# A linear-attention recurrence fused with two MLPs: attention in steps of all eight heads with 64-token chunks

## The chip, the core and the metric

One core of a Trainium2 chip runs the whole program. The metric is the device time of one execution in microseconds, the median of several runs. Engines are named as in the profile: PE is TensorE, DVE is VectorE, ACT is ScalarE, POOL is GpSimd, SP is SyncE, which here only starts DMAs.

## What is computed

A recurrence over 768 tokens with a decaying 48 x 48 state for each of 4 batches and 8 heads, then two MLPs on the 3072 resulting tokens: 384 to 2048 and back, first with an ELU, then with a sigmoid-gated unit.

```python
for t in range(S):                       # B, H, S, D = 4, 8, 768, 48
    cur = np.einsum('bhd,bhe->bhde', u[None] * kt, vt)
    y[:, :, t] = np.einsum('bhd,bhde->bhe', rt, state + cur)
    state = wt[:, :, :, None] * state + np.einsum('bhd,bhe->bhde', kt, vt)
x = y.transpose(0, 2, 1, 3).reshape(B * S, H * D)
h = x @ w_in;  x = where(h > 0, h, exp(min(h, 0)) - 1) @ w_out
h = x @ w2_in; out = (h / (1 + exp(-1.702 * h))) @ w2_out
```

## The kernel before

**The recurrence by levels.** Instead of going token by token, the kernel takes chunks of 128 tokens. Inside a chunk, the score of two tokens needs the product of all decays between them. It is built by halving: at level h (1, 2, 4 ... 64) the right half of each block of 2h tokens in r and the left half in k are multiplied by decays (`update`, lines 545 to 558, DVE), and PE multiplies k by r for the pairs whose nearest common block has that size (`products`, line 748). The decays of blocks come from a tree of products (`tree`, line 528). For small h the matmuls compute 32 x 32 blocks, more than is needed, and DVE picks the wanted entries through masks (`pick`, line 576, L596). The scores of the token with itself come from u*k (here u*r, `near`, line 734). Between chunks there is a state: k is transposed by PE (`turn_products`, L114), multiplied by v (`kv_products`, L127), and DVE carries the state (`state_update`, L154). The outputs y are scores times v (L137) plus state times r (L143), accumulated in PSUM.

**Steps.** A step treats half a sequence (384 tokens, `HALF`) of four heads (`U` = 2 pairs; the two heads of a pair lie on partitions 0 to 47 and 64 to 111). Eight heads, two halves and four batches give 16 steps, indexed (i, x). The end of a step (turning k, states, outputs) is done inside the next step. Everything is double buffered in x.

**The MLP rides.** A group is 384 tokens through one MLP; there are 8 groups for each MLP. A group has 16 hidden tiles of 128, and each tile takes nine matmuls up (`up`, L824) and nine down (`down`, L842), 128 x 128 on 384 columns, because fp32 numbers are split into a high and a low part in fp32r (x_hi, x_lo; g_hi, g_lo; the two halves of a weight tile), and three of the four products are kept. The last 13 of the 16 steps (`LAG` = 3) each carry half a group: eight up blocks, then eight down pieces. After each up block ACT computes relu and exp (L423, L425), DVE the gate (L620), ACT its high part (L429), DVE its low part (L625). The order of the work on every engine is written out by hand in a `step` function for each engine; for PE it alternates:

```python
level(i, x, half, 0, 1, first)      # attention: one level of one pair of heads
mlp(3)                              # MLP: nine matmuls
```

**Data paths.** SP loads r, k, w, u of a step (`load`, line 265), stores y to `y_scratch` in HBM (`store`, L297) and reads a full group of x back from it (`load_x`, L308), which ACT and DVE split (L436, L644). The first six results of the first MLP go to `x2_scratch` in HBM. During the first steps, the weights of MLP 1 arrive through two staging buffers, ACT copies the high part (L416) and POOL computes the low part (L351).

**The second part.** `mlps` (line 874) holds the last step's end, the rest of MLP 1 (one and a half groups) and the 8 groups of MLP 2, in which up and down alternate tile by tile (L1201, L1212). The weights of MLP 2 replace those of MLP 1 tile by tile.

## Time and profile before

| | |
|---|---|
| median of 3 runs | 1101.1 us (1100.88 to 1101.79) |
| the profiled execution | 1101.46 us |
| its span, first to last instruction | 1099.3 us |
| PE / PE weight loads / DVE / ACT / POOL busy | 94% / 87% / 59% / 44% / 7% |
| granted TensorE clock, mean | 0.975 |
| HBM read, written | 39.96 MB, 12.98 MB |

The span is shorter than the time of its execution by what lies around the first and the last instruction. A busy share is that of an engine over the whole span. In the timeline a burst of like instructions is one row with its count, its start and the time from its first start to its last end; a matmul's record lasts longer than the distance to the next one's start, since matmuls overlap. An fp32 matmul leaves two records, an fp32r matmul and a transpose one. The granted clock is a share of 2.4 GHz; 0.5 is 1.2 GHz.

### The profile page before, as it was taken

The page shows a single profiled execution, that of the slowest core. Times are in us where ns is not written, and L with a number is a line of the kernel's source. Part 1 is how long each engine was busy: PE and PEld are TensorE (multiplying, and loading weights), DVE is VectorE, ACT ScalarE, POOL GpSimd, SP SyncE. Part 2 cuts the span into 40 slices and gives each one's busy share as a digit, 9 for nine tenths or more (in the row PEclk, how much of TensorE's full clock was granted, in tenths as well). Part 3 has the DMA queues.
Part 4 walks back from the last instruction along what each step waited for, and adds up shares of the span by engine and source line. Part 5 has one row for each costly group of instructions (what it writes and reads, how often), then busy time and mean ns, then how long its engine had stood idle before and what let it go on. Part 6 is the DMA issues. An engine that isn't in the chain of part 4 may idle for free. (4 is left out here: it accounts for less than half of the span.)

```text
span 1099.3 us, 27196 instructions
## 1 busy us (share of the span) xinstructions
PE 1033.3 (94%) x10912; PEld 951.5 (87%) x10912; DVE 645.0 (59%) x1587; ACT 488.2 (44%) x987; POOL 73.3 (7%) x55
## 2 busy tenths in 40 slices
PE   2658999999899999999999999999999999999998
PEld 1547888888788888788888899999999999999998
DVE  7998677677577687477676543333443434343433
ACT  2445455446246445346444457633333333333332
POOL 5450000000000000000000006400000000000000
PEclk9758999999999999999999999999999999999999
DMA  7453212212212212212210413200000000000000
GB/s 167 106 142 78 49 43 65 56 45 55 58 45 56 56 45 66 46 45 61 51 47 33 146 60 115 73 1 22 1 21 0 21 22 0 21 0 22 1 22 22
DMA packets 24096, 54.56 MB, mean 50 GB/s; under 512 B 3248, under 2 KB 15792, under 8 KB 23984
## 3 DMA queue, kind: packets, MB, share of 16 engines
q1 hardware_dynamic: 22704, 46.66, 16.4%
q0 software_dynamic: 1280, 6.29, 2.0%
q8 instruction: 84, 1.38, 0.6%
q14 instruction: 28, 0.23, 0.1%
HBM read 39.96 MB, written 12.98 MB: 48 GB/s over the span
## 5 line engine op out<-in xcount | busy, mean ns | idle before, releaser
L1201 PE MATMUL psum<-x_hi,w_split 128*128 128x384 f32 x912 | 232.6, 336 | 0.0
L1212 PE MATMUL psum<-g_hi,w_split 128*128 128x384 f32 x912 | 232.6, 336 | 0.0
L842 PE MATMUL psum<-g_hi,w_split 128*128 128x384 f32 x624 | 172.5, 348 | 0.0
L1119 DVE TENSOR_TENSOR gate<-expo,psum 128x384 f32<-128x384 f32 x128 | 70.9, 554 | 160.6 <-ACT expo L1038 160.6
L1201 PEld LDWEIGHTS psum<-x_hi,w_split 128*128 128x128 f32 x912 | 164.9, 188 | 0.0
L1212 PEld LDWEIGHTS psum<-g_hi,w_split 128*128 128x128 f32 x912 | 164.8, 188 | 0.0
L824 PE MATMUL psum<-x_hi,w_split 128*128 128x384 f32 x624 | 161.3, 340 | 0.0
L1201 PE MATMUL psum<-x_lo,w_split 128*128 128x384 f32 x456 | 153.5, 337 | 0.1
L1212 PE MATMUL psum<-g_lo,w_split 128*128 128x384 f32 x456 | 153.3, 336 | 0.0
L1038 ACT ACTIVATE expo<-psum 128x384 f32<-128x384 f32 x128 | 63.0, 492 | 170.4 <-PE psum L1201 170.4
L1125 DVE TENSOR_TENSOR g_lo<-gate,g_hi 128x384 fp32r<-128x384 f32 x152 | 84.9, 559 | 90.2 <-ACT g_hi L1045 90.2
L824 PE MATMUL psum<-x_lo,w_split 128*128 128x384 f32 x312 | 116.7, 374 | 8.2 <-DVE gate L620 6.2
L1045 ACT ACTIVATE g_hi<-gate 128x384 fp32r<-128x384 f32 x152 | 80.1, 527 | 97.9 <-DVE gate L1119 82.4
L556 DVE TENSOR_TENSOR raw<-raw,wtree 128x384 f32<-128x384 f32 x160 | 96.6, 604 | 40.5 <-PE psum L765 32.4
L842 PEld LDWEIGHTS psum<-g_hi,w_split 128*128 128x128 f32 x624 | 111.8, 188 | 5.9 <-issue 2.2
L824 PEld LDWEIGHTS psum<-x_hi,w_split 128*128 128x128 f32 x624 | 115.0, 191 | 0.0
L620 DVE SCALAR_TENSOR_TENSOR gate<-expo,psum 128x384 f32<-128x384 f32 x104 | 57.7, 554 | 86.9 <-ACT expo L425 85.5
L842 PE MATMUL psum<-g_lo,w_split 128*128 128x384 f32 x312 | 107.8, 346 | 0.0
L429 ACT ACTIVATE g_hi<-gate 128x384 fp32r<-128x384 f32 x104 | 54.8, 527 | 84.7 <-DVE gate L620 84.7
L759 PEld LDWEIGHTS psum<-raw 128*32 128x32 f32 (+1 forms) x3840 | 50.1, 115 | 43.6 <-issue 43.6
L1201 PEld LDWEIGHTS psum<-x_lo,w_split 128*128 128x128 f32 x456 | 85.6, 188 | 0.6 <-DVE x_lo L1113 0.4
L1212 PEld LDWEIGHTS psum<-g_lo,w_split 128*128 128x128 f32 x456 | 85.6, 188 | 0.0
(85 smaller groups left out, 1222.5 us busy)
## 6 DMA issues: line engine op xcount, KB each, us to landing
raw<-rkwu_dram SPq DMA_DIRECT2D x32, 288.4 KB, 5.7
staging<-weights_dram POOLq DMA_DIRECT2D x16, 384.0 KB, 3.9
raw<-rkwu_dram SPq DMA_DIRECT2D x32, 144.0 KB, 4.5
v_sb<-v_tokens_dram SPq DMA_DIRECT2D x16, 288.0 KB, 2.8
y_scratch<-y_sb SPq DMA_DIRECT2D x64, 72.0 KB, 1.8
staging<-y_scratch SPq DMA_DIRECT2D x7, 576.0 KB, 4.5
out_dram<-o_sb SPq DMA_DIRECT2D x7, 576.0 KB, 3.0
x_scratch<-x_sb SPq DMA_DIRECT2D x6, 576.0 KB, 3.3
```

The lines of the kernel that those rows point to most:

```text
L429: act.activation(g_hi[:, f, :], gate[:, :], ACT.Copy).then_inc(hi_done, 1)
L556: dve.tensor_tensor(r, r, wr, ALU.mult).then_inc(upd_done, 1)
L620: dve.scalar_tensor_tensor(out=gate[:, :], in0=expo[:, :], scalar=-1.0, in1=mlp_bank(f, x), op0=ALU.add, op1=ALU.max).then_inc(gate_done, 1)
L759: mm = pe.matmul(dst.rearrange("p (a b h) -> p a b h", a=2, h=h), kk[:, o:o + m], right_half(r[:, :, o:o + 32], h), start=True, stop=True)
L824: mm = pe.matmul(mlp_bank(f, x), w_tile((1 - x) * FT + f, lo, kt * P), xx, start=n == 0, stop=n == 3 * KT - 1)
L842: mm = pe.matmul(mlp_bank(FT + m, x), w_tile((1 - x) * FT + f, lo, (KT + m) * P), gg[:, f, :], start=at == 0, stop=at == 3 * FT - 1)
L1038: act.activation(expo[:, f % 2, :], hidden(f), ACT.Sigmoid, scale=1.702).then_inc(exp_done, 1)
L1045: act.activation(g_hi[:, f % 4, :], gate[:, f % 2, :], ACT.Copy).then_inc(hi_done, 1)
L1119: dve.tensor_tensor(gate[:, f % 2, :], expo[:, f % 2, :], hidden(f), ALU.mult).then_inc(gate_done, 1)
L1125: dve.tensor_tensor(g_lo[:, f % 4, :], gate[:, f % 2, :], g_hi[:, f % 4, :].bitcast(F32), ALU.subtract).then_inc(lo_done, 1)
L1201: mm = pe.matmul(hidden(f), w_tile(f, lo, kt * P), xx, start=n == 0, stop=n == 3 * KT - 1)
L1212: mm = pe.matmul(acc(q, m), w_tile(f, lo, (KT + m) * P), gg, start=f == first_tile(g) and n == 0, stop=f == NF - 1 and n == 2)
```

## The change

The attention is written anew, and both parts become one program.

- A step holds all eight heads (`U` = 4 pairs) of half a sequence; there are 8 steps instead of 16. A step's own end (turning, states, outputs) lies in the step itself.
- Chunks have 64 tokens (`CH`), so level 64 goes away and there are 6 chunks in a half instead of 3.
- Each level is one burst on PE for all heads and one pair of updates on DVE (1536 and 768 elements a partition). Only step 0 works in two halves (`grow_pair`).
- The bonus u multiplies k (`bonus`, ACT).
- Keys-values and outputs use 64 rows of the array (a chunk's tokens) or 48, and turn from matmul to matmul through both halves of the rows and of the columns.
- Steps 1 to 7 each carry a full group of MLP 1 (16 tiles), up and down alternating as in the second part. Step 0 carries none. Group 7 of MLP 1 and MLP 2 follow as before.
- x of a group is put together in SBUF (`x_raw`): PSUM goes to it and to `y3` by copies, and six small DMAs from SBUF to SBUF (`fill_gaps`, three on SP, three on POOL) move rows of heads 6 and 7 into the partitions 48 to 63 and 112 to 127. The rows of w_in are reordered on the host to match. `y_scratch` is gone.
- r, k, w and v have one buffer each, the next step's being loaded as soon as this step is through with each. MLP 1's weights use three staging buffers, and DVE computes their low parts in step 0 (`w1_low`); POOL does so only for MLP 2.

```diff
-CH = 128
-U = 2
-LAG = 3
+U = H // 2
+CH = 64
+NC = T // CH
+NB = T // P
...
+                def load_rv(i):
+                    sp.wait_ge(y_done, (i - 1) * N_Y + N_Y)
+                    for a, src in enumerate(of_step(r_dram, i)):
+                        sp.dma_start(arena[64 * a:64 * a + D, a * UT:(a + 1) * UT], src).then_inc(r_in, 16)
+                    sp.dma_start(v_sb[:].rearrange("p c u a e -> p (c u a e)"),
+                                 v_dram[bass.ds(i, 1)].rearrange("o s n -> (o s) n")).then_inc(v_in, 16)
+                def fill_gaps(i):
+                    sp.wait_ge(xc_done, i * N_XC + N_XC)
+                    sp.wait_ge(yc_done, i * N_YC + N_YC)
+                    for m in range(KT):
+                        sp.dma_start(x_raw[48:64, m, :], y3[16 * m:16 * m + 16, 0, :]).then_inc(gap_sp, 16)
...
+                def step(i, stored=None, more=True):
+                    if stored is not None:
+                        store_x2(stored)
+                    if more:
+                        load_w(i + 1)
+                        load_k(i + 1)
+                    fill_gaps(i)
+                    if more:
+                        load_rv(i + 1)
...
+                def load(f):
+                    pool.dma_start(w1_raw[f % NW1], weights1[f]).then_inc(w1_in[f % NW1], 16)
...
+                for f in range(NW1, 11):
+                    pool.wait_ge(wlo_done, f - NW1 + 1)
+                    load(f)
+                fill_gaps(0)
+                for f in range(11, NF):
+                    pool.wait_ge(wlo_done, f - NW1 + 1)
+                    load(f)
+                with pool.Fori(1, STEPS) as i:
+                    fill_gaps(i)
...
+                def update_r(i, k, us):
+                    h = 1 << (k - 1)
+                    d = decay(k, us)
+                    n = d.shape[1]
+                    z = r[:, :, us, :].rearrange("p a u (b two h) -> p a (u b) two h", two=2, h=h)[:, :, :, 1, :]
+                    by = d[:, :, 0:1].rearrange("p (o b) one -> p o b one", o=1).to_broadcast([P, 2, n, h])
+                    return dve.tensor_tensor(z, z, by, ALU.mult)
...
+                def grow_r(i, k):
+                    open_update(i, k, 1)
+                    if k > 1:
+                        dve.wait_ge(upd_done, upd(i, k - 1, 1))
+                    update_r(i, k, ALL).then_inc(upd_done, 1)
+                def grow_k(i, k):
+                    update_k(i, k, ALL).then_inc(upd_done, 1)
+                def grow_pair(k, pair):
+                    open_update(0, k, pair)
+                    if k > 1:
+                        dve.wait_ge(upd_done, upd(0, k - 1, pair))
+                    us = slice(2 * pair, 2 * pair + 2)
+                    update_r(0, k, us)
+                    update_k(0, k, us).then_inc(upd_done, 1)
...
+                def pick(i, h):
+                    k = NEAR.index(h)
+                    dve.wait_ge(lev_done, lev(i, k, 1))
+                    if h == 1:
+                        dve.wait_ge(pick_done, i * N_PICK + 2)
+                    else:
+                        dve.wait_ge(pick_done, i * N_PICK + PICKS[h] - 1)
+                    dve.sem_inc(pick_open, 1)
+                    src = BANKS[(k + 2) % 3][:, 0:384]
+                    m = masks[:, M_OFF[h]:M_OFF[h] + 16].rearrange("p (o b h) -> p o b h", o=1, h=h).to_broadcast(
+                        [P, 24, 16 // h, h])
...
+                def w1_low(f):
+                    dve.wait_ge(whi_done, f + 1)
+                    at = 2 * f * WF
+                    dve.tensor_tensor(w_split[:, at + WF:at + 2 * WF], w1_raw[f % NW1],
+                                      w_split[:, at:at + WF].bitcast(F32), ALU.subtract).then_inc(wlo_done, 1)
...
+                def near(i):
...
+                        if first:
+                            pe.wait_ge(uk_done, 2 * pair + 2)
+                        for u in (2 * pair, 2 * pair + 1):
+                            for c in range(NB):
+                                for j in range(4):
+                                    o = c * P + 32 * j
+                                    at = (u % 2) * 192 + c * 64
+                                    pe.matmul(BANKS[pair][32 * j:32 * j + 32, at:at + 64].rearrange("p (a t) -> p a t", a=2),
+                                              uk[:, u, o:o + 32], r[:, :, u, o:o + 32], start=True, stop=True)
+                        products(1, Z, pair).then_inc(lev_done, 1)
...
+                def products(h, bank, pair):
...
+                                for par in range(2):
+                                    o = c * P + 64 * par
+                                    to = 64 * par + 32 * pair
+                                    mm = pe.matmul(bank[to:to + 32, at:at + 64].rearrange("p (a t) -> p a t", a=2),
+                                                   kk[:, u, o:o + 32], r[:, :, u, o + 32:o + 64], start=True, stop=True)
+                    return mm
+                def level(i, k):
+                    if k < 5:
+                        pe.wait_ge(pick_done, i * N_PICK + k)
+                    else:
+                        pe.wait_ge(pick_done, i * N_PICK + PICKS[4])
+                    split = type(i) is int and i == 0
+                    for pair in range(2):
+                        if split:
+                            pe.wait_ge(upd_done, upd(i, k, pair))
+                        elif pair == 0:
+                            pe.wait_ge(upd_done, upd(i, k, 1))
+                        if split or pair == 0:
+                            pe.sem_inc(level_open, 1)
+                        products(1 << k, BANKS[(k + 2) % 3] if k < 5 else Y, pair).then_inc(lev_done, 1)
...
+                def keys_values(i, half):
+                    def product(c, u, a):
+                        z, slot = PLACE[c]
+                        rows = slice(64 * (c % 2), 64 * (c % 2) + 64)
+                        at = (slot + u) * D
+                        n = (u * NB + c // 2) * P + 64 * a
+                        return pe.matmul(BANKS[z][64 * a:64 * a + 64, at:at + D], kt[rows, n:n + 64],
+                                         v_sb[rows, c // 2, u, a, :], start=True, stop=True)
...
+                    pe.sem_inc(level_open, 1)
+                    for even in (0, 2):
+                        for u in range(U):
+                            for a in range(2):
+                                product(even, u, a)
+                                mm = product(even + 1, u, a)
+                    mm.then_inc(kv_done, 1)
+                    for u in range(U):
+                        for a in range(2):
+                            mm = product(4, u, a)
+                    mm.then_inc(kv_done, 1 + half)
+                    if half == 0:
+                        pe.wait_ge(kv_done, i * N_KV + 2)
+                        pe.sem_inc(level_open, 1)
+                        for u in range(U):
+                            for a in range(2):
+                                mm = product(5, u, a)
+                        mm.then_inc(kv_done, 1)
...
+                def outputs(b, i, half):
+                    def place(c, u, a):
+                        z, slot = PLACE[c]
+                        to = 64 * (a ^ (u % 2))
+                        at = (slot + u) * CH
+                        return BANKS[z][to:to + D, at:at + CH]
+                    def from_scores(c, u, a):
+                        rows = slice(64 * (c % 2), 64 * (c % 2) + 64)
+                        return pe.matmul(place(c, u, a), v_sb[rows, c // 2, u, a, :], scores[rows, u, c // 2, a, :],
+                                         start=c in (0, 1, 4) and u == 0, stop=False, skip_group_check=True)
+                    def from_state(c, u, a):
+                        rows = slice(64 * a, 64 * a + D)
+                        return pe.matmul(place(c, u, a), state[rows, (c - 1) % NC, u, :],
+                                         r[rows, a, u, c * CH:(c + 1) * CH], start=False, stop=True, skip_group_check=True)
+                    pe.wait_ge(asm_done, i * N_ASM + N_ASM)
+                    pe.wait_ge(state_done, states_before(b, half) + N_STATE[half])
+                    pe.sem_inc(level_open, 1)
+                    for n, pair in enumerate(((4, 1), (0, 3), (2, 5))):
+                        if n == 2:
+                            pe.wait_ge(y_done, i * N_Y + 1)
+                            pe.sem_inc(level_open, 1)
+                        for u in range(U):
+                            for a in range(2):
+                                for c in pair:
+                                    mm = from_scores(c, u, a)
+                        if n != 1:
+                            mm.then_inc(y_done, 1)
+                    for n, (even, odd) in enumerate((((0, 2), (1, 3)), ((4, 5), (0, 2)), ((1, 3), (4, 5)))):
+                        pe.wait_ge(y_done, i * N_Y + 2 + n)
+                        pe.sem_inc(level_open, 1)
+                        for u in range(0, U, 2):
+                            for z in range(2):
+                                for c, uu in ((even[z], u), (odd[z], u + 1)):
+                                    if half == 1 or c > 0:
+                                        for a in range(2):
+                                            mm = from_state(c, uu, a)
+                        mm.then_inc(y_done, 1)
...
+                def step(b, i, half, g, q, more=True):
+                    def unit_up(f):
+                        if f + 2 < NF:
+                            up(g, q, f + 2)
+                        else:
+                            up(g + 1, 1 - q, f + 2 - NF)
+                    def unit_down(f):
+                        down(g, f, 0, freed=f == 0 and (type(g) is not int or g > 0))
+                    def unit(f):
+                        unit_up(f)
+                        unit_down(f)
+                    unit_up(0)
+                    level(i, 1)
+                    unit_down(0)
+                    unit(1)
+                    level(i, 2)
+                    unit(2)
+                    unit_up(3)
+                    level(i, 3)
+                    unit_down(3)
+                    unit(4)
+                    level(i, 4)
+                    unit(5)
+                    unit_up(6)
+                    level(i, 5)
+                    unit_down(6)
+                    unit(7)
+                    turn(i)
+                    unit(8)
+                    unit_up(9)
+                    keys_values(i, half)
+                    unit_down(9)
+                    unit(10)
+                    unit_up(11)
+                    outputs(b, i, half)
+                    unit_down(11)
+                    unit(12)
+                    unit(13)
+                    unit(14)
+                    if more:
+                        near(i + 1)
+                    unit(15)
```

On PE, around a level of a riding step before (`raw` holds r and k):

```order
L824 MATMUL psum<-x_hi,w_split 128x384 x2
L759 MATMUL psum<-raw 32x32 x12
L824 MATMUL psum<-x_lo,w_split 128x384
L824 MATMUL psum<-x_hi,w_split 128x384 x2
L824 MATMUL psum<-x_lo,w_split 128x384
L824 MATMUL psum<-x_hi,w_split 128x384 x2
L824 MATMUL psum<-x_lo,w_split 128x384
L824 MATMUL psum<-x_hi,w_split 128x384 x2
L114 MATMUL psum<-ident,k_fin 128x128 x3
L759 MATMUL psum<-raw 32x32 x12
```

and now (`arena` holds r and k, and more):

```order
L964 MATMUL psum<-x_lo,w_split 128x384
L964 MATMUL psum<-x_hi,w_split 128x384 x2
L832 MATMUL psum<-arena 32x32 x48
L977 MATMUL psum<-g_lo,w_split 128x384
L977 MATMUL psum<-g_hi,w_split 128x384 x2
L977 MATMUL psum<-g_lo,w_split 128x384
L977 MATMUL psum<-g_hi,w_split 128x384 x2
L977 MATMUL psum<-g_lo,w_split 128x384
```

Before, 12 matmuls of one pair of heads stand behind a block of nine MLP matmuls; now 48 of all heads stand in one piece, with 18 to 27 MLP matmuls to the next level.

On DVE, in a riding step, before (`raw<-raw,wtree` are updates, `gate` and `g_lo` the MLP's, `scores<-diag` the end of the step before):

```order
L620 SCALAR_TENSOR_TENSOR gate<-expo,psum 128x384
L556 TENSOR_TENSOR raw<-raw,wtree_2 128x192x2
L558 TENSOR_TENSOR raw<-raw,wtree_2 128x96x2
L625 TENSOR_TENSOR g_lo<-gate,g_hi 128x384
L603 COPY scores<-diag 32x6x32 x4
L620 SCALAR_TENSOR_TENSOR gate<-expo,psum 128x384
L154 SCALAR_TENSOR_TENSOR state<-state,wchunk,psum 128x48 x4
L556 TENSOR_TENSOR raw<-raw,wtree_4 128x96x4
```

and now, from the update of level 3 to the update of level 4 (shapes are strided, 384x4 and 192x8 both make 1536 elements with the two heads):

```order
L533 TENSOR_TENSOR arena<-arena 128x384x4
L627 SCALAR_TENSOR_TENSOR gate<-expo,psum 128x384
L539 TENSOR_TENSOR arena<-arena 128x192x4
L632 TENSOR_TENSOR g_lo<-gate,g_hi 128x384
L584 COPY_PREDICATED blocks<-masks,psum 128x384
L627 SCALAR_TENSOR_TENSOR gate<-expo,psum 128x384
L533 TENSOR_TENSOR arena<-arena 128x192x8
L632 TENSOR_TENSOR g_lo<-gate,g_hi 128x384
```

The picks, which stood together at the end of a step, now stand between the levels, one behind each update of k, and the levels after them wait for them.

On SP, in a step of before with its x:

```order
L279 DMA raw<-rkwu_dram 48x2x384
L281 DMA raw<-rkwu_dram 48x1538
L279 DMA raw<-rkwu_dram 48x2x384
L281 DMA raw<-rkwu_dram 48x1538
L297 DMA y_scratch<-y_sb 48x384 x4
L285 DMA v_sb<-v_tokens_dram 128x576
L308 DMA staging<-y_scratch 128x3x384
```

and now:

```order
L171 DMA arena<-w_channels_dram 48x1536 x2
L171 DMA arena<-k_channels_dram 48x1536 x2
L198 DMA x_raw<-y 16x384 x3
L189 DMA arena<-r_channels_dram 48x1536 x2
L190 DMA v_sb<-v_tokens_dram 128x1152
```

The loads of r and v stand behind the three DMAs that fill x_raw, and those behind the loads of w and k.

## Rows read from the trace of the kernel before

**Rows 1.** The page: parts 1 and 2, busy time and the 40 slices.
```profile
PE 1033.3 (94%) x10912; PEld 951.5 (87%) x10912; DVE 645.0 (59%) x1587; ACT 488.2 (44%) x987; POOL 73.3 (7%) x55
...
PE   2658999999899999999999999999999999999998
```

**Rows 2.** The windows: busy us (instructions) of each engine, granted clock, DMA share, GB/s.
```profile
0.00:95.00 95.00, 47.03 (x1116) 37.27 (x1117) 83.10 (x183) 35.31 (x64) 43.13 (x39) 0.75 0.54 133
95.00:615.30 520.30, 505.38 (x6994) 435.28 (x6994) 368.63 (x1059) 257.47 (x557) 0.00 (x0) 0.99 0.22 51
3.00:13.00 10.00, 0.00 (x0) 0.00 (x0) 4.35 (x7) 0.95 (x2) 1.97 (x3) 1.00 0.93 217
298.00:299.00 1.00, 1.00 (x8) 1.00 (x5) 0.54 (x2) 0.00 (x0) 0.00 (x0) 0.73 0.07 16
```

**Rows 3.** The chain of waits, last stage: start us, length us, what.
```profile
893.26 1.57 PE psum L1201 x9
```

**Rows 4.** The timeline of PE, riding steps: start us, length us, engine, line, what, count.
```profile
134.33 0.54 PE L744 MATMUL psum<-ur,raw 128*32 128x64 f32 x24
134.69 0.37 PE L759 MATMUL psum<-raw 128*32 128x32 f32 x24
134.99 0.45 PE L824 MATMUL psum<-x_lo,w_split 128*128 128x384 f32 x1
...
303.55 0.45 PE L824 MATMUL psum<-x_lo,w_split 128*128 128x384 f32 x1
...
305.26 0.49 PE L114 MATMUL psum<-ident,k_fin 128*128 128x128 f32 x3
...
312.57 0.86 PE L137 MATMUL psum<-scores,v_sb 128*48 128x128 f32 x12
313.37 0.86 PE L143 MATMUL psum<-r_fin,state 48*48 48x128 f32 x12
...
324.92 0.53 PE L765 MATMUL psum<-raw 128*32 128x64 f32 x12
325.38 0.44 PE L842 MATMUL psum<-g_hi,w_split 128*128 128x384 f32 x1
```

**Rows 5.** The timeline of PE before the riding steps, at half clock.
```profile
86.23 0.81 PE L759 MATMUL psum<-raw 128*32 128x32 f32 x48
```

**Rows 6.** The timeline of PE: a step's first row, and the loop's edge.
```profile
251.67 0.54 PE L744 MATMUL psum<-ur,raw 128*32 128x64 f32 x24
...
292.56 0.54 PE L744 MATMUL psum<-ur,raw 128*32 128x64 f32 x24 [1.09 <-issue]
...
297.45 0.36 PE L744 MATMUL psum<-ur,raw 128*32 128x64 f32 x10 [2.03 <-issue]
```

**Rows 7.** The timeline of DVE in a riding step.
```profile
107.00 0.55 DVE L556 TENSOR_TENSOR raw<-raw,wtree 128x384 f32<-128x384 f32 x1
107.47 0.35 DVE L558 TENSOR_TENSOR raw<-raw,wtree 128x192 f32<-128x192 f32 x1
107.74 0.55 DVE L625 TENSOR_TENSOR g_lo<-gate,g_hi 128x384 fp32r<-128x384 f32 x1
```

**Rows 8.** The DMA issues: KB each, median us from issue to landing.
```profile
raw<-rkwu_dram SPq DMA_DIRECT2D x32, 288.4 KB, 5.7
staging<-weights_dram POOLq DMA_DIRECT2D x16, 384.0 KB, 3.9
...
y_scratch<-y_sb SPq DMA_DIRECT2D x64, 72.0 KB, 1.8
```

**Rows 9.** The waits of PE: us in total, times, longest us.
```profile
PE psum L824 <- DVE gate L620: 6.2, 12, 0.6
...
PE psum L824 <- DVE x_lo L644: 2.0, 6, 0.4
```

**Rows 10.** The timeline of DVE and POOL in the start.
```profile
22.10 2.03 POOL L351 TENSOR_TENSOR w_split<-staging,w_split 128x768 fp32r<-128x768 f32 x1 [2.72 <-ACT w_split L416]
...
22.37 2.17 DVE L556 TENSOR_TENSOR raw<-raw,wtree 128x384 f32<-128x384 f32 x1
```

1700 lines of the change are left out of this document (707 added, 993 removed).

## Prediction

> **What bounds the kernel now.** I read the page first [rows 1]: PE is busy for 94% of the span, its loads for 87%, DVE for 59%. Only the first four of the 40 slices fall short on PE; from the fifth on every digit but the last is 9. So the time is what PE has to do, plus the start. The windows divide it [rows 2]: 95.0 us before the first MLP matmul (PE busy 47.0 of them, granted clock 0.75), 520.3 us in which MLP and attention share PE, and the last 484.0 us of MLP. In the last stage the chain of waits consists of PE pieces, nine matmuls in 1.56 to 1.57 us [rows 3]: 0.1737 us for one, and no engine is waited for. All 4608 MLP matmuls (16 groups, 16 tiles, 18 each) come to 4608 x 0.1737 = 800.4 us. They are the same in both kernels, so only 1099.3 - 800.4 = 298.9 us can be argued about: the start, the attention's own matmuls, waits and the two ends.
>
> The timeline of a riding step gives the rates [rows 4]. Every fp32 matmul leaves two records, so L744's 12 matmuls stand as x24. From the start of a burst to the next: L744 0.36 us; L759 0.30; L137 0.80; L765 0.46. The MLP block behind a burst runs from 303.55 to 305.26, 1.71 us where 1.56 would do: re-entry costs 0.15. The L759 burst of 134.69 ends at 135.06 and one record lasts 0.205 (mean), so its last start is 134.86: 24 starts in 0.17 us, 7 ns each, and the other 0.14 of its 0.30 is draining. A burst is thus about 0.15 fixed, plus columns: L744 (64 columns, four column groups at once) 13 to 15 ns a record; L765 (64 columns, two groups) (0.46 - 0.15)/12 = 26; L137 (128 columns, two groups) (0.80 - 0.15)/12 = 54. All fit one rule: time goes with columns and falls with the number of groups at work. At half clock, 48 records of L759 take 0.81 [rows 5], (0.81 - 0.205)/47 = 13 ns, twice as much.
>
> **The riding steps.** Three steps of before lie between the L744 bursts at 134.33 and 251.67 [rows 4, 6]: 39.1 us each, 25.0 of it MLP; two of them, 78.2 us, do what one new step does. The new step has 288 MLP matmuls, 50.0 us, and these bursts:
> near, 48 matmuls of L744's kind and 48 of L759's: 96 x 14 + 96 x 8 ns + 0.15 = 2.3 us. Levels 1 to 4, 96 records at 8 ns + 0.15 = 0.92 each, 3.7. Level 5 (32 x 64, two groups): 48 x 26 ns + 0.15 = 1.4. Level 6 of before (L769) is gone, since chunks are 64 tokens. Twelve transposes of 128 columns, one record each, 54 ns: 0.8. Keys and values, 40 or 48 matmuls of 48 columns: 20 ns a record with two groups, by L765's rate; here both halves of the rows and of the columns are used in turn, 10 ns if four quadrants work at once: 1.3 with the second wait. Outputs, 88 to 96 matmuls of 64 columns: 184 x 13 ns + five waits for its own last result at 0.25 = 3.7. Re-entry nine times, where before has some 34 in two steps: 1.35. Sum 14.6.
> Four quadrants at once is a choice: no row of before shows it (L143 uses two, on the diagonal, at L137's pace). I take it since the rate went down with each further part of the array in use. The other bound is two, 20 and 27 ns: 3.4 us more a step. The Trainium skill, TensorEngine Tiling (Array Packing), Available Configurations, lists 64x64 as four independent tiles; that would be my value, and no run here shows it yet.
>
> Waits. DVE costs come from start to start [rows 7]: 128x384 0.47, 128x192 0.27, so about 0.06 + 1.07 ns an element; the 1536-element update 1.7, its k part 0.88, together 2.6 a level for all heads. A pick of 384 I put at the same 0.5. A step holds 16 x 0.95 for the gates, 15.5 for updates, 3.5 for picks, 4.4 for states, 1.3 for the split and 4 of the rest: 44 of 67 us. It fits, but each level has its own deadline. Laying both orders against each other, with elu 1.1 us after `up` and a level 0.92: level 3 waits for pick(1) (DVE through at 16.6 us, PE there at 16.2) 0.4; level 5 for pick(4) 0.4; transposes for pick(16) 0.35; outputs for the last states 0.5. The rest of the MLP hides the remainder, 1.5 to 2 units of 3.13 us between levels. `up` of the next group waits for x_lo: after the outputs come the copies 0.9, DMAs from SBUF to SBUF (y_scratch's 72 KB landed in 1.8 [rows 8]; POOL takes 0.56 to issue one), ACT's split 1.15, DVE's tree and split 3.3: 8.8 us, against five MLP blocks, 7.8: 1.0. r of the next step, queued on SP behind the gap DMAs, lands some 8 us after the outputs (5.7 [rows 8]), and `near` comes after 11: hidden, by 3 us. Together 2.75, all after waits that before had too (gate 6.2 us in 12, x_lo 2.0 in 6 [rows 9]). Between nothing and 6 us a step is possible.
> A step: 50.0 + 14.6 + 2.75 = 67.4, against 78.2.
>
> **The start.** Before's is bound by DVE, and by POOL beside it: when POOL splits a weight tile (2.03 us), one DVE operation of 0.55 lasts 2.17 [rows 10]; 16 such tiles cost DVE some 26 us. Now DVE does that work itself, 16 x 0.86 = 13.8, and POOL computes nothing. But only one step runs ahead of the MLP, not three. By the clock: 217 GB/s flowed from 3 to 13 us [rows 2], so 1.8 MB of k, r, w is there at 13; tree 2.5; six levels of two pairs 24 with picks, three weight tiles and waits, 39.7. Then the weights bind: three buffers, a reload 0.56 + 3.9 [rows 8] + 0.84 on ACT: w1_low(7) ends at 50.6; states 55.2; outputs at half clock 61.7; copies, gaps, and r with v behind them 69.7; near 3.8 at half clock, updates and split 77.4; the last eight weight tiles through three buffers, two reload rounds deep, 91.5. `up(0, 2)` starts at about 92. The y_scratch round trips go; they were hidden, and I cost them at nothing.
>
> **The sum.** 92 + 4590 x 0.1737 (797.3; 18 matmuls are done before) + 7 x 14.6 less one near (99.8) + 7 x 2.75 (19.3) + one loop edge + 2 for the clock after PE's idle time + 3.5 at the end. The edge: at before's, PE idles 1.09 and again 2.03 us in the midst of L744, with nothing to wait for, and the granted clock is 0.73 in the microsecond behind [rows 2, 6]; two steps grow by 5.4. The new loop has one such edge. 1019.3 us of span. The profiled execution took 1101.46 for a span of 1099.3, 2.2 more, and the median is 0.4 below it: 1021.
>
> **Rivals.** (A) **Two quadrants only**: 7 x 3.4 = 24 more, 1045. For it: before never has row halves at work in one column group. Chance 0.17.
> (B) **Small matmuls keep a price**: a level costs four times its old piece, 1.28, and near 2.64, since nothing longer than 48 records of this kind is in the trace; the 7 ns could be a queue filled beforehand. 4 x 0.36 + 0.5 = 1.9 a step, 13 in all; with A, 1058. Against it: the 48 records at half clock kept half the rate [rows 5]. The Trainium skill, the same page, Instruction Overhead, says a matmul has about 60 cycles of overhead, so that one of few columns lasts as long as one of 60. By that, L759 would cost what L744 does, 14 ns, and a level 1.5: 1036. The rows speak against it (7 ns against 13 to 15). Chance 0.10, A's part aside.
> (C) **DVE's deadlines**: all six levels, kv, outputs and near each 0.7 us later: 6.3 a step, 44 in all, 1065. For it: bursts cannot start before all heads' updates are through, where before's first pair hid the second's. Against: 44 of 67 us busy. Chance 0.10.
> (D) **Slower: instructions run short.** A burst of near is 384 instructions (records and their loads) in 2.2 us, outputs 370 in 3.7; before's longest is 96 at that rate. Where PE ran dry behind the loop edge it lost 2.03 us, and with the clock's drop 3.7 in that step. If that happens in bursts as such: 63 bursts; from 22 of them on (80/3.7) the kernel is slower than before; in half of them 32 x 3.7 = 118, 1139. Against it: 18 MLP matmuls, 36 instructions in 3.13 us, stand between most bursts and leave the fetch time, and PE shows no such hole away from the loop's edge [rows 1]. Chance 0.05.
> (E) **No change in what matters**: the new step has 460 attention matmuls for two times 197, so with A, B and C together PE gains nothing from bursts: 78 a step, 7 x 10.6 = 74 more, 1095. Chance 0.03; half of that within 0.2%.
>
> **The numbers.** The forecast, 1021, has 0.55. A, B, C reach to 1065. The start may be 8 us off to either side, the stalls nothing (19 less): about 1000 below. Range 1000 to 1062 leaves out D, E, and a little of C and of the lower end. A measurement here tells 0.2% from no change. Faster 0.93, within 0.2% 0.02, slower 0.05.
>
> **What would show it.** Right: near to near in a steady step 66 to 69 us; a level of 96 records in 0.8 to 1.0; outputs 3.5 to 4; `up(0, 2)` at 85 to 98; DVE operations in the start at their own length; PE idle before levels 3 and 5 under 1 us each. Wrong: level bursts of 1.3 (B), outputs above 5.5 (A), idle time of PE put down to issue inside bursts (D), or PE waiting for DVE more than 5 us a step (C).

## The result, and the profile after

The changed kernel takes 1057.6 us (median of four runs, 1055.5 to 1058.4) where the kernel before takes 1101.2: ratio 0.9601, 95% interval 0.9586 to 0.9616. It is faster, inside the range of 1000 to 1062, and 36.6 us slower than the forecast of 1021. The profiled execution took 1057.42 with a span of 1055.4, so the 2.0 us around the span are as assumed (2.2), and the miss lies in the span: 1055.4 against 1019.3. One execution of a kernel further down, that with seven staging buffers, took 1568.7 us at a granted clock of 0.56, and is left out of that kernel's ratio as slow.

The page of the changed kernel, parts 1 and 2, answers to [rows 1]:

```profile
PE 953.0 (90%) x11872; PEld 922.3 (87%) x11872; DVE 546.2 (52%) x894; ACT 456.8 (43%) x859; POOL 56.5 (5%) x65
...
PE   2434999998998988999999999999999999999998
```

PE is 80 us less busy (1033.3 before), although it executes more instructions, and its share fell from 94% to 90%. The work shrank as meant; what the forecast lacked is in idle time. Four slices of the riding steps show an 8. The windows cut the span where the terms of the sum end (columns as in rows 2: busy us and count of PE, PE's loads, DVE, ACT, POOL; clock; DMA share; GB/s):

```profile
0.00:101.48 101.48, 35.47 (x1119) 32.09 (x1119) 54.24 (x83) 29.23 (x45) 16.23 (x28) 0.97 0.45 118
101.48:530.92 429.44, 398.84 (x6966) 375.30 (x6966) 269.10 (x430) 214.27 (x413) 8.68 (x18) 0.99 0.18 43
530.92:1055.40 524.48, 518.67 (x3789) 514.94 (x3788) 222.85 (x382) 213.34 (x402) 31.62 (x19) 1.00 0.09 32
```

`up(0, 2)` starts at 101.48 and not at 92: 9.5 of the 36.1 us. Behind it come 953.9 us instead of 927.3: 26.6 more, some 23 of them before 530.92, where PE is idle for 30.6 us, and the rest in the seventh riding step behind it. The waits of PE between 102 and 560 us, and the one that is over by 101.48 (us in total, times, longest):

```profile
PE psum L964 <- DVE gate L627: 11.4, 2, 10.3
PE psum L964 <- DVE x_lo L614: 8.0, 6, 1.5
PE psum L832 <- DVE blocks L584: 6.9, 7, 1.0
PE psum L964 <- issue: 3.8, 5, 0.9
PE psum L841 <- DVE blocks L584: 3.3, 6, 0.6
PE psum L977 <- issue: 2.1, 2, 1.0
...
PE psum L832 <- issue: 1.4, 2, 0.8
PE psum L872 <- DVE blocks L584: 1.3, 6, 0.2
```

Two kinds stand there: DVE's deadlines (x_lo, and the picks of L584), some 19.5 us; and 7.3 us of "issue" in L964, L977 and L832, for which the forecast had 5.4 at one loop edge.

One straight step, the one whose `near` starts at 460.28, from PE's timeline, answers to [rows 4]:

```profile
460.28 0.88 PE L819 MATMUL psum<-arena 128*32 128x64 f32 x48
...
486.22 1.02 PE L832 MATMUL psum<-arena 128*16 128x32 f32 x96
...
492.63 0.58 PE L841 MATMUL psum<-arena 128*32 128x64 f32 x14 [0.49 <-DVE blocks L584]
...
498.72 0.60 PE L872 MATMUL psum<-ident,arena 128*128 128x128 f32 x4
499.54 0.66 PE L872 MATMUL psum<-ident,arena 128*128 128x128 f32 x4 [0.22 <-DVE blocks L584]
...
505.27 1.61 PE L884 MATMUL psum<-v_sb,arena 64*64 64x48 f32 x80
...
507.63 0.44 PE L977 MATMUL psum<-g_lo,w_split 128*128 128x384 f32 x1
...
514.26 1.56 PE L918 MATMUL psum<-blocks,v_sb 64*48 64x64 f32 x96
516.01 1.45 PE L923 MATMUL psum<-arena,state 48*48 48x64 f32 x48 [0.19 <-PE psum L918]
...
518.24 0.44 PE L977 MATMUL psum<-g_lo,w_split 128*128 128x384 f32 x1
...
527.60 0.44 PE L964 MATMUL psum<-x_lo,w_split 128*128 128x384 f32 x1 [1.25 <-DVE x_lo L614]
...
530.92 0.77 PE L819 MATMUL psum<-arena 128*32 128x64 f32 x40
```

It takes 70.64 us; 67.4 was forecast. From start to start, less the waits, beside the forecast's terms: `near` 2.31 (2.3); levels 1 to 4, of which L832 at 486.22 is one (0.95), 3.94 (3.7); level 5 1.28 (1.4); transposes 1.45 (0.8); keys and values 507.63 - 505.27 = 2.36 (1.3); outputs 3.98 (3.7); the MLP's own 50.0. The blocks of 27 MLP matmuls between the bursts last 4.8 to 4.9 us where 27 x 0.1737 is 4.69, so re-entries come to 2.4 (1.35); waits 0.93, 0.49, 0.22 and 1.25, together 2.9 (2.75, whose own five terms make 2.65). The excesses, 0.24 - 0.12 + 0.65 + 1.06 + 0.28 + 1.05 + 0.15, make 3.3, which is the miss (3.24 from start to start) but for rounding.

That step is in straight code behind PE's loop. The loop's own four start at 167.76, 238.88, 312.58 and 386.72 and took 71.12, 73.70, 74.14 and 73.56: three of the four are 3 us longer. In the first of these three PE's timeline has three holes in the midst of MLP pieces:

```profile
243.10 0.62 PE L964 MATMUL psum<-x_hi,w_split 128*128 128x384 f32 x2 [0.95 <-issue]
...
250.48 0.34 PE L977 MATMUL psum<-g_hi,w_split 128*128 128x384 f32 x1 [1.04 <-issue]
...
265.17 0.51 PE L964 MATMUL psum<-x_hi,w_split 128*128 128x384 f32 x2 [0.76 <-issue]
```

The same three matmuls of the loop's second pass, 147.7 us later, have holes of 0.77, 1.04 and 0.77.

Ratios below are to the kernel before, run on the same chip; where an experiment is compared with the changed kernel, it is by the difference of its ratio to 0.9601, times 1101.2 us. With the intervals of the ratios, such a difference is good to some 3 to 4 us either way, so the bursts and waits in the timelines are read beside it.

### The profile page after: what moved, and what is told of

The parts are those of the page before. It is cut to its first block, busy times and chain, and to the rows that moved or that the text cites. A ratio compares the mean times of both kernels' runs of the same rounds, so it can differ in the third digit from the quotient of the medians.

```text
span 1055.4 us, 27022 instructions
## 1 busy us (share of the span) xinstructions
PE 953.0 (90%) x11872; PEld 922.3 (87%) x11872; DVE 546.2 (52%) x894; ACT 456.8 (43%) x859; POOL 56.5 (5%) x65
## 3 DMA queue, kind: packets, MB, share of 16 engines
q1 hardware_dynamic: 12448, 38.74, 13.5%
q8 instruction: 87, 1.43, 0.6%
## 4 chain that ended last, share of the span: by engine, by line
PE 79%; DVE 7%; issue 3%; ACT 3%; DMA 1%; SPq 0%; DVEq 0%; POOL 0%; POOLq 0%
PE psum L964 36%; PE psum L977 33%; PE psum L832 3%; ACT expo L363 1%; PE psum L923 1%; DVE blocks L584 1%; ACT expo L361 1%; DVE arena L515 1%; PE psum L884 1%; PE psum L819 1%; PE psum L918 1%; DVE gate L627 1%; DVE arena L539 1%; PE psum L841 1%; DVE x_lo L614 1%
## 5 line engine op out<-in xcount | busy, mean ns | idle before, releaser
L964 PE MATMUL psum<-x_hi,w_split 128*128 128x384 f32 x1536 | 396.1, 339 | 3.2 <-issue 3.2
L977 PE MATMUL psum<-g_hi,w_split 128*128 128x384 f32 x1536 | 391.3, 336 | 2.1 <-issue 2.1
L964 PE MATMUL psum<-x_lo,w_split 128*128 128x384 f32 x768 | 264.8, 345 | 24.1 <-DVE x_lo L614 12.0
L964 PEld LDWEIGHTS psum<-x_hi,w_split 128*128 128x128 f32 x1536 | 281.9, 189 | 5.1 <-issue 4.9
L977 PEld LDWEIGHTS psum<-g_hi,w_split 128*128 128x128 f32 x1536 | 277.0, 188 | 0.0
L977 PE MATMUL psum<-g_lo,w_split 128*128 128x384 f32 x768 | 261.0, 340 | 0.0
L632 DVE TENSOR_TENSOR g_lo<-gate,g_hi 128x384 fp32r<-128x384 f32 x256 | 142.7, 557 | 122.5 <-ACT g_hi L372 121.8
L964 PEld LDWEIGHTS psum<-x_lo,w_split 128*128 128x128 f32 x768 | 144.9, 189 | 27.3 <-DVE w_split L653 10.6
L977 PEld LDWEIGHTS psum<-g_lo,w_split 128*128 128x128 f32 x768 | 144.3, 188 | 4.6 <-issue 2.4
L368 ACT ACTIVATE expo<-psum 128x384 f32<-128x384 f32 x128 | 63.0, 492 | 172.8 <-PE psum L964 172.8
L361 ACT ACTIVATE expo<-psum 128x384 f32<-128x384 f32 x128 | 62.5, 488 | 165.5 <-PE psum L964 165.2
L533 DVE TENSOR_TENSOR arena<-arena 128x1536 f32<-128x1536 f32 (+1 forms) x54 | 85.2, 1578 | 15.1 <-PE psum L832 12.1
L832 PEld LDWEIGHTS psum<-arena 128*32 128x32 f32 (+1 forms) x3840 | 43.0, 114 | 33.4 <-issue 33.4
L832 PE MATMUL psum<-arena 128*32 128x32 f32 (+1 forms) x3840 | 48.0, 206 | 24.9 <-DVE blocks L584 11.9
L363 ACT ACTIVATE expo<-expo 128x384 f32<-128x384 f32 x128 | 67.3, 526 | 4.1
L539 DVE TENSOR_TENSOR arena<-arena 128x768 f32<-128x768 f32 (+1 forms) x54 | 46.6, 863 | 0.0
L819 PE MATMUL psum<-arena 128*32 128x64 f32 x768 | 16.6, 243 | 21.3 <-DMA ident<-ident_dram 12.3
```

The lines of the kernel that those rows point to most:

```text
L361: act.activation(expo[:, f % 2, :], hidden(f), ACT.Relu, scale=-1.0).then_inc(neg_done, 1)
L363: act.activation(expo[:, f % 2, :], expo[:, f % 2, :], ACT.Exp, scale=-1.0).then_inc(exp_done, 1)
L368: act.activation(expo[:, f % 2, :], hidden(f), ACT.Sigmoid, scale=1.702).then_inc(exp_done, 1)
L533: return dve.tensor_tensor(z, z, by, ALU.mult)
L539: return dve.tensor_tensor(z, z, d[:, :, 1:2].to_broadcast([P, d.shape[1], h]), ALU.mult)
L632: dve.tensor_tensor(g_lo[:, f % 4, :], gate[:, f % 2, :], g_hi[:, f % 4, :].bitcast(F32), ALU.subtract).then_inc(lo_done, 1)
```

## Experiments

### The split of x ahead of the tree

```diff
                     gate_lo(g, 14)
+                    split(g + 1, 1 - q)
                     if more:
                         for m in range(1, 6):
                             tree(i + 1, m)
-                    split(g + 1, 1 - q)
```

> DVE splits x for the next group before it multiplies up the tree of the next step (five small products, 1.6 us), instead of behind it. Theory (the wait for x_lo is DVE's order, nothing else): in the changed kernel's static step x_hi is there at 524.95, DVE works on the tree until 526.20 and ends the split at 527.50, while the up matmuls wait 1.25 us until 527.60; with the split first it ends about 1.2 us earlier, the wait of L964 for x_lo (12.0 us in 7) falls below 3 us, and the kernel takes 1057.6 - 7 x 1.2 = 1049 us (1048 to 1051). Rival (the chain to x_hi through the copies, the gap DMAs and ACT is what is late): x_hi moves nothing, the wait stays above 1 us a step, the time stays within 2 us of 1057.6. Second rival (the tree is late next): near or level 1 waits for the tree or for the updates instead, and less than half of the gain is left, 1053 or more.

1050.3 us, ratio 0.9533 [0.9505, 0.9562]: 7.5 us less. The wait for x_lo, 12.0 us in 7 before, is no longer among the first in PE's list, and in the steps 0.4 and 0.8 us of it are left in two. The wait was the order of DVE's program: the tree for the next step stood ahead of the split (until 526.28 in the step above), although the first update of that step came only at 533.34. Neither rival holds.

### Seven staging buffers in the start

```diff
+        w1_raw += [state (its first 768 columns), x_raw (likewise), expo, gate]
-                for f in range(6):
+                for f in range(10):
                     w1_high(f)
                 off32(0, 0)
...
                     kt_copy(0, z)
+                for f in range(10, 12):
+                    w1_high(f)
                 for j in range(4):
                     assemble(0, j)
...
-                for f in range(3, 8):
+                for f in range(5, 12):
                     w1_low(f)
                 states(0, 0, 0, range(6))
+                for f in range(12, NF):
+                    w1_low(f)
```

(The first line is told in words; `w1_low` 0 to 4 stand behind the first five picks, and none is left behind near(1).)

> The start alone: seven staging buffers for the weight tiles instead of three (state, x_raw, expo and gate are idle then), and the low parts are computed as far as possible in DVE's idle time, the last four before the output copies; nothing is split behind near(1). Theory (the weights bind the start, as the prediction had it, and the prediction missed their order on ACT): the states no longer wait 5.5 us behind L385 (start at 52 to 54.5 instead of 56.2), the stretch from the split of x (86.2) to the first gate (100.8) falls to the two up pieces, and up(0, 2), which starts at 101.5, starts at 86 to 89: the kernel takes 1057.6 - 13.5 = 1044 us (1042 to 1047). Rival (the loads themselves bind, 6.3 MB at some 217 GB/s, and delay k, r and v or the near stage): tiles still arrive after 60 us, up(0, 2) at 95 or later, 1051 us or more.

1044.4 us, ratio 0.9478 [0.9442, 0.9513]: 13.5 us less. The two up pieces follow the split at once, from this row of PE's timeline on:

```profile
84.60 0.69 PE L968 MATMUL psum<-x_lo,w_split 128*128 128x384 f32 x1 [4.01 <-DVE x_lo L614]
```

They take 5.9 us, at half clock, and `up(0, 2)` starts at 90.52: later than the 86 to 89 expected, and 11.0 us earlier than in the changed kernel. The other 2 us come behind it: the changed kernel's first piece took 3.15 us and its level 1 1.44, at a granted clock of 0.50 after 10.3 us of idle time, and here they take 1.79 and 0.99. near(1) starts at 74.55 instead of 76.55. The states start 0.9 us earlier (55.26 for 56.18), since they no longer stand behind L385, although a hole of PE of 2.79 us, put down to issue, made keys and values 1.8 us later. The rest of the 2.0 is in the outputs, whose state part took 2.9 us instead of 3.8. So the weights bound the end of the start, as the forecast said, and cost more than it said.

### The first MLP pieces ahead of near(1)

```diff
-                near(1)
                 for f in range(2):
                     up(0, 0, f)
+                near(1)
```

and on DVE split(0, 0) ahead of pick_diag(1, 0), on SP `load_rv(1)` ahead of `fill_gaps(0)`; the buffers as before.

> As the kernel with seven staging buffers, and besides the first group's MLP does not wait for near(1): PE does up(0, 0) and up(0, 1) first, DVE splits x before it picks and updates, and SP asks for r and v of step 1 before the gap DMAs. Theory: x_hi is there at 73.15 and DVE idles from 68.3 to 80.6 in the changed kernel, so x_lo is there at 74.4 or earlier, the two up pieces run while r is still in flight, near(1) follows and up(0, 2) starts at 79 to 83; level 1 of the step then waits 1 to 2 us for the updates. Against the kernel with only the buffers another 5 us: 1039 us (1037 to 1042), that is 18.5 below the changed kernel. Rival (near(1) has to be paid in the same place anyway, since r comes when it comes and the updates behind it are late for level 1): level 1 waits 4 us or more, and at most 2 us are won over the buffers alone.

1043.5 us, ratio 0.9482 [0.9457, 0.9507]: no different from the buffers alone, where 5 us were expected. The timelines of ACT show why, of the run with the buffers alone first, then of this one:

```profile
70.15 1.16 ACT L347 ACTIVATE x_hi<-x_raw 128x1152 fp32r<-128x1152 f32 x1 [1.80 <-DMA x_raw<-y]
```

```profile
74.81 1.16 ACT L349 ACTIVATE x_hi<-x_raw 128x1152 fp32r<-128x1152 f32 x1 [6.79 <-DMA x_raw<-y]
```

SP issued its gap DMAs at 66.69 us here and at 66.59 without this change, so it is their landing that is late: they are small, and stood behind r and v, which SP now asked for first. x_hi came 4.7 us later. Neither theory nor rival had this. Even so `up(0, 2)` starts at 86.32 instead of 90.52; of these 4.2 us only 1.3 are left at the next `near` (153.47 for 154.76), since PE idled before level 1 and ran there at a granted clock of 0.50 (88 to 90 us). And PE has a hole put down to issue in near(1), and two smaller ones behind it:

```profile
86.07 0.32 PE L839 MATMUL psum<-arena 128*32 128x32 f32 x10 [1.74 <-issue]
```

### PE's loop written out

```diff
-                with pe.Fori(1, B - 1) as b:
+                for b in range(1, B - 1):
                     step(b, b * 2, 0, b * 2 - 1, 1)
                     step(b, b * 2 + 1, 1, b * 2, 0)
```

(on PE alone)

> PE's loop over the riding steps is written out (steps 2 to 5 straight behind each other, on PE alone), nothing else changes. In the changed kernel the looped steps take 73.7, 74.1 and 73.6 us and the straight ones 71.1 and 70.6, with holes of PE of 0.6 to 1.1 us put down to issue that lie 256 or 512 instructions apart. Theory L (the holes belong to the loop: its registers, or its jumping back): in the written-out version all steps take 70.6 to 71.2, and the kernel 1057.6 - 4 x 2.8 = 1046 us (1045 to 1049). Theory F (a fetched packet of 256 instructions costs PE up to 1 us wherever it meets a queue that a burst has emptied, looped or not): the holes stay, at other places, the steps stay at 73 to 74 and the time within 3 us of 1057.6.

1050.7 us, ratio 0.9540 [0.9514, 0.9566]: 6.7 us less. The steps take 70.8, 70.1, 72.3, 70.4 and 72.5 us. Between 102 and 600 us PE's waits for issue in the up and down pieces are gone, and what is left lies in `near` (and 0.4 in the outputs):

```profile
PE psum L832 <- issue: 3.1, 2, 1.6
```

The size speaks for theory L, but the two holes of 1.5 and 1.6 us are in straight code, which only theory F has; the changed kernel has such a hole, too, outside its loop (0.59 us at 535.14). The shifted program, below, takes this up.

### The order of the array's quarters: diagonal neighbours

```diff
                                 product(even, u, a)
-                                mm = product(even + 1, u, a)
+                                mm = product(even + 1, u, 1 - a)
...
-                                for c in pair:
-                                    mm = from_scores(c, u, a)
+                                for n2, c in enumerate(pair):
+                                    mm = from_scores(c, u, a ^ n2)
```

> Only the order of products inside two bursts changes: in keys-values and in the score part of the outputs, two neighbouring matmuls now use diagonal quarters of the array (rows 0-63 with columns 0-63, then rows 64-127 with columns 64-127, and so on), where before two neighbours used both row halves in the same column half. Theory (four quarters work at once only if neighbours share neither rows nor columns; the state part of the outputs already has that order and runs at 0.60 us for 32 records): L884's 64-record burst falls from 1.77 to about 1.1 us, L918's 96 records from 1.75 to about 1.45, 0.9 us a step and the kernel by 6 to 7 us, to 1051 (1049 to 1053). Rival A of the prediction (at most two work at once, in whatever order): no burst moves by more than 0.1 us, the time stays within 1.5 us of 1057.6.

1057.3 us, ratio 0.9619 [0.9594, 0.9644]: the same. L884's first burst takes 1.76 us, L918's 1.75, both as before to 0.01. The order of the quarters makes no difference where both row halves and both column halves are in turn within four neighbours anyway.

### Two quarters only

```diff
-                        for u in range(0, U, 2):
-                            for z in range(2):
-                                for c, uu in ((even[z], u), (odd[z], u + 1)):
+                        for par in range(2):
+                            for u in range(0, U, 2):
+                                for z in range(2):
+                                    c, uu = ((even[z], u), (odd[z], u + 1))[par]
```

> The counterpart: in the state part of the outputs all products of the even heads come first and then all of the odd ones, so that within a stretch only two diagonal quarters alternate. Theory (four at once): L923's 32-record pieces go from 0.60 to about 1.0 us (27 ns a record, the two-group rate of L765 before), three pieces a step, +1.0 to 1.5 us a step and 7 to 10 us in all, 1066 (1064 to 1069). Rival (two at once is all there is, and the 14 ns come from elsewhere): no change, within 1.5 us of 1057.6.

1059.8 us, ratio 0.9647 [0.9620, 0.9675]: 5 us more than the changed kernel, 2.5 more than the run before it on the same chip. The intervals of these two runs overlap, so the bursts have to show it. PE's timeline, same step:

```profile
517.74 0.93 PE L923 MATMUL psum<-arena,state 48*48 48x64 f32 x32 [0.17 <-PE psum L923]
518.60 0.45 PE L978 MATMUL psum<-g_lo,w_split 128*128 128x384 f32 x1
```

The last piece took 0.60 us, (0.60 - 0.15)/32 = 14 ns a record; now 0.86, 22 ns. More than two quarters do work at once; the rival, which is A of the prediction, falls. The cost is 0.33 us in this step, whose other two pieces have 24 records and hardly grow, and 0.76 in a step with three pieces of 32 (in the first, the pieces start 1.08 us apart instead of 0.83), not 1.0 to 1.5: two quarters are not as slow as the 26 ns of L765 [rows 4]. The Trainium skill, TensorEngine Tiling (Array Packing), Available Configurations, has four independent 64x64 tiles: this pair of runs agrees, with 14 against 22 ns, a factor of 1.6 and not of 2.

### Three picks earlier

```diff
-                    gate_lo(g, 4)
                     pick(i, 1)
+                    gate_lo(g, 4)
...
-                    gate_lo(g, 7)
                     pick(i, 4)
+                    gate_lo(g, 7)
...
-                    gated(g, 9)
                     pick(i, 16)
+                    gated(g, 9)
```

> DVE does three picks (1, 4 and 16) one operation of 0.55 us earlier, in front of the gate's low part or of the gate. In the changed kernel PE waits for them 0.93 us before level 3, 0.49 before level 5 and 0.22 before the transposes of every step. Theory (these waits are DVE's order, each level has its own deadline and there is slack behind it): the waits fall to 0.4, 0 and 0, 1.2 us a step, and the kernel to 1057.6 - 7 x 1.2 = 1049 us (1048 to 1052). Rival (the time comes back: the gates that are pushed back hold up the next up or down piece, since DVE is as late there): the waits for L584 go, but waits for the gate or for g_lo of similar size appear, and the time stays within 2 us of 1057.6.

1047.7 us, ratio 0.9535 [0.9511, 0.9560]: 7.3 us less than the changed kernel, 9 less than the run with diagonal neighbours on the same chip. PE's waits between 440 and 520 us: the picks' are down to one of 0.5, that of level 3, and those before level 5 and the transposes are gone. The list begins with

```profile
PE psum L964 <- DVE x_lo L614: 2.6, 2, 1.3
```

The gates that were pushed back hold nothing up. These waits, too, were places in DVE's program, at a load of 52%.

### Two bursts per level again

```diff
                         products(1 << k, ...).then_inc(lev_done, 1)
+                        if pair == 0 and between is not None:
+                            between()
...
-                    level(i, 1)
-                    unit_down(0)
+                    level(i, 1, lambda: unit_down(0))
```

and likewise in levels 2 to 5, with an up or a down piece between the pairs.

> The one-burst-per-level part undone: in each of the five levels the first head pair's burst is followed by an MLP piece of 9 matmuls (1.56 us) and only then comes the second pair's. Theory (a burst has a fixed price: 0.15 us of draining and some 0.2 us of re-entry into the MLP, as the prediction costs it): 5 x 0.35 = 1.75 us a step more, 12 us in all; and since each level's updates wait for the second pair, they come 1.56 us later, which the deadlines of levels 3 and 5, already missed by 0.93 and 0.49, pass on: up to another 1.5 us at each, 1057.6 + 12 + 7 x 3 = 1091 at most, 1078 (1070 to 1091) as the expectation. Rival (bursts cost only their columns; what the change won is the chunk size and the missing level 6, not the number of bursts): less than 5 us more, 1062 or below.

1090.5 us, ratio 0.9928 [0.9904, 0.9952]: 36 us more, where 33 was the most expected. So with this order on DVE, one burst per level instead of two is worth most of the 43.6 us which the whole change brings. PE's timeline of level 3 in the same step:

```profile
503.60 0.63 PE L832 MATMUL psum<-arena 128*32 128x32 f32 x48 [1.32 <-DVE blocks L584]
504.17 0.45 PE L979 MATMUL psum<-g_lo,w_split 128*128 128x384 f32 x1
...
505.93 0.63 PE L832 MATMUL psum<-arena 128*32 128x32 f32 x48
506.49 0.44 PE L966 MATMUL psum<-x_lo,w_split 128*128 128x384 f32 x1
```

Two bursts take 0.57 + 0.56 = 1.13 us for the 0.98 of one, and a down piece between them 1.76 where 9 x 0.1737 is 1.56: 0.35 for one more burst, as expected before this run; the forecast's own terms, 0.15 and 0.15, make 0.30. Over the step, which takes 75.67 us, 5.0 more, the bursts' price is 1.75. Most of the rest is waits for picks, 4.2 us in this step where the changed kernel has 1.6; 0.3 is a hole. The price of a burst is the smaller part; the larger one is that updates and picks of a level wait for its last pair. An order of DVE's program that suits two bursts was not tried, and might take back part of it.

### PE's program shifted by 128 instructions

```diff
                 pe.wait_ge(cleared_p, 4)
+                for _ in range(128):
+                    pe.sem_inc(shifted, 1)
                 near(0)
```

> 128 empty semaphore instructions are put ahead of PE's first matmul, where PE waits for data anyway; everything behind them stands 128 instructions later in PE's program, half of a 16 KB piece of instructions. The written-out loop removed most of the holes (four steps 9 us shorter in the loop's part), but two of 1.5 and 1.6 us came up in straight steps, and in the changed kernel the holes at 243.10, 250.48 and 265.17 lie 256 and 512 PE instructions apart. Theory F (a hole is the passing from one 16 KB piece of PE's program to the next, seen where a burst has emptied the queue): every hole of the riding part moves by 128 instructions, so that those of the changed kernel are gone from their places (2 matmuls into an up piece behind near; 1 into a down piece) and others stand half way between, and by size they come to more or less than 9.8 us as they fall behind bursts or not. Theory L (they belong to certain places of the looped program, its waits against registers): they stay at the same matmuls within the step.

One run, 1078.1 us. near(0) starts at 32.55 us instead of 12.26: 128 empty semaphore instructions took 20.3 us, 0.16 each. Without that the time is 1057.8, the changed kernel's. The holes have moved: none in the step from 257.45, where three were; now one right at the end of the `near` of the next step, and in the step from 476.05, straight code that had none:

```profile
331.79 0.26 PE L833 MATMUL psum<-arena 128*32 128x32 f32 x4 [1.98 <-issue]
...
480.06 0.26 PE L833 MATMUL psum<-arena 128*32 128x32 f32 x4 [1.66 <-issue]
...
488.42 0.41 PE L978 MATMUL psum<-g_lo,w_split 128*128 128x384 f32 x1 [2.22 <-issue]
```

The windows from one hole of the changed kernel to the next count the loads of PE (the second column's count):

```profile
243.10:250.48 7.38, 5.90 (x125) 1.00 0.19 72
250.48:265.17 14.69, 12.08 (x252) 1.00 0.23 48
```

With as many matmuls, that is 249 and 504 instructions, besides the few for semaphores, which the windows do not count. Between the changed kernel's holes at 322.59 and 329.29, inside two level bursts, it is 252, between the two of this run at 480.06 and 488.42 it is 254, and between two of the combined kernel below, in straight code, 509. The page counts 87 instruction packets for 1.43 MB, 16 KB each. Holes that keep a distance of 256 instructions and that move when the program is shifted belong to the passing from one packet to the next: theory F. (That 256 instructions of PE are one such packet is inferred; the page does not say which engine's a packet is.) It does not say why the written-out loop had fewer; that version also drops the loop's own instructions (26,855 in all instead of 27,022), so that its passings fall elsewhere. Whether the loop costs anything besides is open.

### The widths of the two sides

```diff
-                    return pe.matmul(BANKS[z][64 * a:64 * a + 64, at:at + D], kt[rows, n:n + 64],
+                    return pe.matmul(BANKS[z][64 * a:64 * a + 32, at:at + D], kt[rows, n:n + 32],
...
-                        return pe.matmul(place(c, u, a), v_sb[...], scores[rows, u, c // 2, a, :],
+                        return pe.matmul(place(c, u, a)[:, 0:32], v_sb[...], scores[rows, u, c // 2, a, 0:32],
```

> A measurement of rates; it leaves part of the computation out: keys-values takes 32 of the 64 columns of the transposed k (its stationary side), so half of each product's rows is missing, and the score part of the outputs takes 32 of the 64 tokens of the scores (its moving side). In the changed kernel L884 runs at (1.77 - 0.15)/80 = 20 ns a record with 64 stationary and 48 moving columns, L918 at (1.75 - 0.15)/96 = 17 ns with 48 stationary and 64 moving, L832 at 7 to 8 ns with 32 and 32; their order did not matter. Theory W (with four quarters, and neighbours that differ in all, it is the loading of the stationary side, one after the other, that sets the pace): L884's burst of 80 records falls from 1.77 to 0.95 us, L918's stays at 1.75. Theory M (moving columns set it): L884's stays at 1.77, L918's falls to 0.95.

This kernel leaves out half of each product that it narrows, so only its bursts are read and not its time. One run.

```profile
502.41 1.22 PE L884 MATMUL psum<-v_sb,arena 64*32 64x48 f32 x80
...
510.87 1.32 PE L918 MATMUL psum<-blocks,v_sb 64*48 64x32 f32 x96
```

L884's burst went from 1.77 to 1.37 us, 20 to 15 ns a record, L918's from 1.75 to 1.51, 17 to 14 ns. Neither theory is right: each side has a part, and with either of them halved a record still costs 14 to 15 ns, as L923's do. What sets this floor, which L832's 8 ns are below, stays open.

### What helped, together

The edits of the first, second, third (with the gap DMAs ahead of r and v again), fourth and seventh experiment, and pick 1 ahead of the gate, too.

> What helped, together: the split of x ahead of the tree (7.3 us alone), the three picks earlier, pick 1 now also ahead of the gate (9.9 alone, some 3 more), PE's loop written out (6.9), seven weight buffers (13 to 14) and the first group's first two up pieces ahead of near(1), but now with SP's gap DMAs ahead of the loads of r and v (in the run before, the gap DMAs waited behind them, x_hi came at 74.8 to 76.0 instead of 70.2 to 71.3; first up expected at 73 to 75 instead of 77.4, worth 3 us). If the gains add, since each lies in another stall: 1057.6 - 7.3 - 12 - 6.9 - 17 = 1014 us (1010 to 1019). Rival (the gains overlap: a later wait of the same step takes up part of each): 1022 or more, with waits for gate, x_lo or updates above 1 us a step.

1011.7 us (1011.4 to 1016.5), ratio 0.9206 [0.9183, 0.9228], 43.5 us less than the changed kernel, and the fastest so far together with the next. The gains add: run singly, four of them made 35.0 us (7.5, 13.5, 6.7, 7.3), and the other 8.5 fall to what was not run by itself, the up pieces with the gap DMAs in front, and pick 1 ahead of the gate. They were not told apart. PE's waits between 100 and 560 us:

```profile
PE psum L837 <- issue: 3.1, 2, 1.6
PE psum L928 <- PE psum L928: 1.9, 11, 0.2
```

Behind these two stand only three more of the same kinds, 0.5 to 1.3 us each: no other engine is waited for any more. Three steps take 67.6, 67.0 and 67.2 us, those with a hole 69.2 and 69.4. The first up piece starts at 72.24.

### Without the empty semaphore instructions

```diff
-                        if split or pair == 0:
-                            pe.sem_inc(level_open, 1)
```

and the same on PE in `near`, `keys_values` and `outputs`, from the combined kernel.

> The combined kernel of the run before, and PE's empty semaphore instructions, one or more ahead of each burst (11 to 12 a step), are left out; the waits then hang on the first matmul itself. In the shifted kernel 128 such instructions moved near(0) from 12.3 to 32.6 us, 0.16 us each. Theory S (the fixed price of a burst, about 0.15 us, and part of the re-entry, is this instruction): each burst loses 0.1 to 0.16 us, levels go from 0.98 to 0.85, the outputs' waits for PE's own results shrink by as much; a step 1.2 to 1.9 us shorter and the kernel, 1011.7 us before, at 1001 (998 to 1004). Rival D (the price is the draining of the array and the fetch of data, and PE's sequencer runs ahead of the array, so that such an instruction in mid-stream is hidden): levels stay at 0.95 or more and the time within 3 us of 1011.7. Holes at passings of 256 instructions may fall elsewhere in both cases, worth up to 3 us either way.

1011.5 us, ratio 0.9194 [0.9179, 0.9208]: as the combined kernel. A level, of the combined kernel and of this one:

```profile
359.62 1.06 PE L837 MATMUL psum<-arena 128*32 128x32 f32 x96
360.61 0.45 PE L982 MATMUL psum<-g_lo,w_split 128*128 128x384 f32 x1
```

```profile
425.82 1.06 PE L836 MATMUL psum<-arena 128*32 128x32 f32 x96
426.80 0.45 PE L974 MATMUL psum<-g_lo,w_split 128*128 128x384 f32 x1
```

0.99 and 0.98 us: rival D's outcome holds. In mid-stream such an instruction costs nothing that shows; only in the start, with nothing else to do, did it show its 0.16 us. That PE's sequencer runs ahead there is rival D's reason, and no run tests it by itself.

## Why the prediction was right, and 36 us too low

**What bounds the kernel**: right. PE's own work and the start make the time, and the change acted on both. The range was kept by 4 us, and in part by luck: its top was set for rivals A, B and C, and other things filled it. Of the signs named beforehand, a step of 66 to 69 us and `up(0, 2)` at 85 to 98 were missed (70.64 and 101.48), the levels, the outputs and the waits before level 5 came as named, those before level 3 touched 1.02 us, and the sign for D came, too: holes inside level bursts, of 0.82 us at 322.59 and 0.59 at 329.29.

**Rates of small matmuls**: right for the bulk. A level of 96 records takes 0.95 to 1.02 us (0.92 forecast), `near` 2.31 (2.3). Rival B, a kept price of 1.28 a level, is out. By the Trainium skill's TensorEngine Tiling (Array Packing), Instruction Overhead, a level would take 1.5, an estimate by that rule with L744's 14 ns a record; the trace has 0.95 to 1.02, and does not agree. The prediction's 1036 for that case leaves `near` out, whose 96 short records would take 6 ns more each, 4 us in all.

**Transposes, keys and values**: the two terms of a burst that were mis-sized. "Twelve transposes of 128 columns, one record each, 54 ns: 0.8" measured 1.45, and 1.23 in one piece once the wait in its midst was gone, so (1.23 - 0.15)/12 = 90 ns. The forecast took L137's pace, of two column groups, for matmuls that use the whole array. The trace of the kernel before had the right one: its three transposes at 305.26 [rows 4] are followed by this row, 0.42 us later, and (0.42 - 0.15)/3 is 90 ns.

```profile
305.68 0.40 PE L759 MATMUL psum<-raw 128*32 128x32 f32 x24
```

As for keys and values, "10 ns if four quadrants work at once: 1.3" measured 20 ns, 2.36. Four quarters are real for the outputs (14 against 22 ns), which came to 3.98 for 3.7, but the rate does not halve again: the widths run shows a part for each side and 14 ns below which neither took it. Rival A, two quarters, is wrong for the outputs, right in size for keys and values alone. 1.7 us a step, 12 in all.

**Re-entry** was 0.15 nine times; the blocks between bursts show 0.2 and more, 1.05 a step, 7 in all. The two-burst run gives the price of a further burst, 0.35, where the forecast's terms make 0.30.

**Waits**: 2.75 forecast, 2.9 measured, in the places named: level 3, level 5, transposes, x_lo. Sizes within: 0.93 for 0.4, 0.49 for 0.4, 0.22 for 0.35, nothing for the states, 1.25 for 1.0. Rival C is out. What the forecast took as the price of the design was the order of a few DVE operations: four operations moved in it took away 2.4 us of the 2.9.

**The loop's edge and rival D**: mis-named. The prediction read every digit of [rows 1] from the fifth to the last but one as 9; the eleventh, with the loop's edge, is an 8. The forecast put one edge at 5.4 us and gave D, instructions running short in bursts, 0.05. The edge at 318 us cost about 2.5 (an idle time of 1.09 and the two holes above), and holes of 0.6 to 1.1 make three of the four looped steps 3 us longer, 9 us in all. D's mechanism is at work, at passings of 256 instructions, of which the riding part's 13,900 matmuls and loads [the window from 101.48 to 530.92] have some 55. Eight of them show up to there, with 0.6 to 1.1 us each; D needed 22 at 3.7.

**The start**: right in what binds its end, 9.5 us short. DVE was through with the six levels and their picks at 46.3 us and not at 39.7: its tree began at 14.73 instead of 13, and it waited for PE's bursts seven times, 5.2 us in all, once behind a hole of PE of 1.80 us put down to issue. Then "w1_low(7) ends at 50.6" came at 56.2. In front of it DVE waited 5.5 us for tiles 6 and 7, which stand on ACT behind the assembly (until 53.5), and the states stand behind them. Not all of this is the order on ACT: the states also need keys and values, which were there at 53.1, so without it they could have started 3 us earlier and no more. r landed at 76.5 instead of 69.7; near(1) had a hole of 1.5 us; and from there the tail of the weights took 14.6 us, 14.1 forecast. DVE's operations had their own length beside an idle POOL, as forecast.

The outputs and `near` did run at half clock, as assumed. The scores' burst of the outputs took 2.81 us, where it takes 1.56 in the steps. The granted clock of the profile does not show it: it is 1.00 from 60 to 70 us, and in the run with two bursts per level, where the same burst lasts as long, 0.50. These are the burst and the window, first of the changed kernel, then of that run:

```profile
60.61 2.81 PE L918 MATMUL psum<-blocks,v_sb 64*48 64x64 f32 x96 [6.25 <-issue]
60.00:70.00 10.00, 6.38 (x176) 5.56 (x176) 3.67 (x10) 3.92 (x9) 1.03 (x3) 1.00 0.02 4
```

```profile
60.66 2.81 PE L920 MATMUL psum<-blocks,v_sb 64*48 64x64 f32 x96 [6.53 <-issue]
60.00:70.00 10.00, 6.38 (x176) 5.56 (x176) 3.71 (x10) 3.88 (x9) 0.98 (x3) 0.50 0.02 6
```

Nor does the mean clock sort the times: other runs of the changed kernel with a lower one took no longer (1055.5 us at 0.961, 1057.4 at 0.995).

**The sum of it**: 9.5 for the start, 7 x 3.2 = 22.4 for the steps and 9 for the holes of looped steps, the edge among them, less the 5.4 forecast for the edge: 35.5 of the 36.1. The 2 us forecast for the clock came: the first up piece took 3.15 us instead of 1.56 and the level behind it 1.44 instead of 0.99, at a granted clock of 0.50 from 100 to 106 us.

## What to carry to other kernels

When a dependent stage rides on a dense one, give it few long bursts, above all because the other engine's work for a level can start only behind its last burst: splitting each level in two cost 36 us, a third of it for the bursts and about half for the waits behind them. Then read each remaining wait of the bound engine as a place in the releasing engine's program: an engine at 52% load was late at four places in each step, and moving four operations was worth 15 us. On a queue shared by a small urgent DMA and large ones, the small one goes first.

## What the runs showed of the hardware that was not expected

- Holes of 0.6 to 2.2 us in PE, at distances of 249, 504, 252, 254 and 509 matmuls and loads, that is, one or two 16 KB packets of instructions, and they move when the program is shifted. In the changed kernel each of the eight before 530.92 lies inside a burst or at most 3 us behind one (a `near` uses up 384 instructions in some 2.3 us). Behind 535.14 PE has none.
- An empty semaphore instruction on PE takes 0.16 us if PE has nothing else to do, and nothing that shows in mid-stream.
- Small DMAs inside SBUF that are issued behind r and v (0.6 MB each) land 4.7 us later.
- A 128 x 128 fp32 transpose in a burst takes some 90 ns, in both kernels.
- The granted clock of a window can be 1.00 over bursts that last as long as in another run at 0.50. The length of a burst that stands in both tells the pace; why the figure differs is open.
